# The inverse of a delta-rule scan: multiplied into keys and values per chunk, or inside each scan step

## The reference

```python
k_n = k / (norm(k) + 1e-6); state = 0
for t in range(S):
    y[t] = q[t] @ state
    state = state + beta[t] * outer(k_n[t], v[t] - k_n[t] @ state)
```

## Time and profile before

| | |
|---|---|
| time, median of 3 runs | 1041.93 us (1041.87 to 1047.24) |
| profiled execution: its own time | 1037.31 us |
| its span | 1035.6 us |
| TensorE busy with matmuls | 979.5 us (95%) |
| VectorE busy | 449.3 us (43%) |
| ScalarE busy | 167.2 us (16%) |
| GpSimd busy | 109.6 us (11%) |
| mean DMA rate | 71 GB/s |

### The profile page before, as it was taken

How to read it: one execution, slowest core, us unless ns; L and a number is a source line. 1 busy time by engine, 2 the same in 40 slices (tenths; PEclk the granted TensorE clock), 3 DMA queues, 4 the chain that set the end, 5 groups by cost and what they waited for, 6 DMA issues and landing times. The chain is left out here.

```text
span 1035.6 us, 22935 instructions
## 1 busy us (share of the span) xinstructions
PE 979.5 (95%) x10037; PEld 661.4 (64%) x10037; DVE 449.3 (43%) x1086; ACT 167.2 (16%) x352; POOL 109.6 (11%) x137
## 2 busy tenths in 40 slices
PE   6989999999999999999999999999999359999996
PEld 5875666566566566557666665666555248788785
DVE  6866753947356835734772565211011212112121
ACT  2121121120121022012102210211110011111110
POOL 4010100011010110001011001001001112212221
PEclk9989999999999999999999999999999769999998
DMA  9502003001300310040022000001900014444400
GB/s 354 234 21 89 3 17 138 2 3 35 120 3 2 108 48 2 1 154 3 1 52 104 3 1 32 18 1 18 373 22 16 32 26 158 151 158 152 153 30 27
DMA packets 29147, 74.03 MB, mean 71 GB/s; under 512 B 3944, under 2 KB 19992, under 8 KB 28160
## 3 DMA queue, kind: packets, MB, share of 16 engines
q1 hardware_dynamic: 18960, 56.74, 15.4%
q10 hardware_dynamic: 6912, 9.55, 2.6%
q0 software_dynamic: 3184, 6.39, 2.0%
HBM read 60.62 MB, written 13.00 MB: 71 GB/s over the span
## 5 line engine op out<-in xcount | busy, mean ns | idle before, releaser
L859 PE MATMUL ps<-xT,wg 128*128 128x384 f32 x576 | 208.3, 499 | 0.7 <-ACT xT L661 0.7
L879 PE MATMUL ps<-wo,prod 128*128 128x393 f32 x576 | 203.4, 501 | 2.9 <-DVE prod L558 2.9
L868 PE MATMUL ps<-xT,wv 128*128 128x384 f32 x576 | 204.6, 491 | 0.0
L558 DVE TENSOR_TENSOR prod<-sig,ps 128x384 f32<-128x384 f32 x96 | 53.2, 554 | 250.3 <-PE ps L868 249.9
L859 PEld LDWEIGHTS ps<-xT,wg 128*128 128x128 f32 x576 | 108.2, 193 | 72.0 <-issue 4.2
L879 PEld LDWEIGHTS ps<-wo,prod 128*128 128x128 f32 x576 | 105.3, 189 | 75.2 <-DVE prod L558 5.3
L868 PEld LDWEIGHTS ps<-xT,wv 128*128 128x128 f32 x576 | 107.0, 190 | 70.8 <-issue 1.3
L1131 PEld LDWEIGHTS ps_h<-xgT,arena 128*128 128x128 f32 x816 | 96.3, 196 | 5.2 <-ACT xgT L1088 1.0
L1131 PE MATMUL ps_h<-xgT,arena 128*128 128x128 f32 x816 | 96.6, 280 | 0.6 <-ACT xgT L1088 0.6
L666 ACT ACTIVATE sig<-ps 128x384 f32<-128x384 f32 x96 | 47.1, 490 | 277.1 <-PE ps L859 277.1
L1143 PE MATMUL ps_y<-arena,hT 128*128 128x384 f32 x272 | 90.5, 486 | 0.0
(11 more groups left out here) (154 smaller groups left out, 775.7 us busy)
## 6 DMA issues: line engine op xcount, KB each, us to landing
arena<-in_moe_w SPq DMA_DIRECT2D x16, 1536.0 KB, 10.6
arena<-in_kq SPq DMA_DIRECT2D x7, 1536.0 KB, 9.8
x_scratch<-x ACTq DMA_DIRECT2D x24, 196.5 KB, 4.1
arena<-in_kr SPq DMA_DIRECT2D x8, 576.0 KB, 5.3
vr<-in_v SPq DMA_DIRECT2D x8, 576.0 KB, 10.6
out<-x ACTq DMA_DIRECT2D x24, 192.0 KB, 3.2
prod<-in_turned_moe_w_out SPq DMA_DIRECT2D x1, 2304.0 KB, 11.6
wo<-in_moe_w_out SPq DMA_DIRECT2D x1, 2304.0 KB, 24.1
```

The costliest lines, as they stand in the source:

```text
L558: nc.vector.tensor_tensor(prod[:, f, :], sig[:, f % 2, :], ps_m[3 - f % 2][:, 0:CT], ALU.mult)\
L859: last = nc.tensor.matmul(ps_m[f % 2][:, 0:CT], wg[:, a, f * P:(f + 1) * P], xT[:, a, :], start=(a == 0), stop=(a == KT - 1))
L868: last = nc.tensor.matmul(ps_m[3 - f % 2][:, 0:CT], wv[:, a, f * P:(f + 1) * P], xT[:, a, :], start=(a == 0), stop=(a == KT - 1))
L879: last = nc.tensor.matmul(ps_m[t][:, 0:XW], prod[:, a, t * P:(t + 1) * P], wo[:, a, :], start=(a == 0), stop=(a == NF - 1))
```

## The change

`wu` is gone with its two evacuations. Each scan step gets a third event `apply` between `read` and `write`: `read` multiplies the bare keys with the state, VectorE takes z = V - K S in place (`z_of`), `apply` multiplies u = T z (16 matmuls of 48 columns), ScalarE copies u to a buffer `ub`, and `write` reads `ub`. The head blocks are laid so that `apply`, `write` and the query part of `gram` cross the partition halves and use all four tiles. The query part of y no longer shares PSUM columns with the score part: ScalarE copies it to `yo` after `read`, and VectorE adds the score part to `yo` after `write`. `gram` is split into 32 matmuls of 64 columns per third in place of 16 of 128.

The squares of the keys get a load of their own (`kn`, 576 KB per chunk, issued for chunk q once `from_lanes` of q - 1 is done). The first root is taken on ScalarE with four short VectorE instructions that refine it; the others stay on GpSimd. The set-up of masks is in another order, and TensorE no longer waits for it at its start. The order by hand has other fill: one dense piece more ahead of `off` 0 where preparation was still under way, `norm` of the next chunk after `off` 1, and in the prologue other `warm` counts and a later start of chunk 1's preparation.

```diff
         order += [("router", 0, 0)] + [("gram", 1, i) for i in range(3)] + [("warm", 0, 14)]     # 12 before
-    order += [("from_lanes", 0, 0), ("router_copy", 0, 0), ("off", 0, 0), ("warm", 1, 4), ("off", 0, 1)]
-    order += [("pt", 0, i) for i in range(3)] + [("warm", 1, 3), ("wu", 0, 0), ("norm", 1, 0), ("warm", 1, 2), ("wu", 0, 1),
-                                                 ("warm", 1, 2)]
-    later = prepare(1)
+    order += [("from_lanes", 0, 0), ("router_copy", 0, 0), ("off", 0, 0), ("warm", 1, 2)] + [("pt", 0, i) for i in range(3)]
+    order += [("off", 0, 1), ("norm", 1, 0), ("warm", 1, 2)]
     for step in scan(0):
+        if step[0:2] == ("apply", 1):
+            later = prepare(1)
         order.append(step)
         if step != scan(0)[-1]:
             order.append(("warm", 1, 1))
-        behind(0.5)
+        behind(0.3)
...
+            late = len(later) > 0
             while later:
                 dense(1.0)
             order.append(("from_lanes", q, 0))
-            dense(2.0)
+            dense(3.0 if late else 2.0)
             order.append(("off", q, 0))
-            if follows:
-                order.append(("norm", q + 1, 0))
             dense(1.2)
             order.append(("off", q, 1))
             dense(1.1)
-            order.append(("wu", q, 0))
-            dense(1.0)
-            order.append(("wu", q, 1))
-            dense(1.0)
             if follows:
-                order += [("gram", q + 1, 0), ("gram", q + 1, 1), ("pt", q + 1, 0)]
+                order += [("norm", q + 1, 0), ("gram", q + 1, 0), ("gram", q + 1, 1), ("pt", q + 1, 0)]
...
             elif stage == "read":                                      # VectorE
-                nc.vector.tensor_tensor(u, u, ps_a[:, 0:2, 0:W4], ALU.subtract).then_inc(u_ready, 1)
+                nc.vector.tensor_tensor(z, z, ps_a[:, 0:2, 0:W4], ALU.subtract).then_inc(z_ready, 1)
+            elif stage == "write":
+                ...  # st as before, from ps_a[:, 0:2]
+                if s % SB:
+                    dve.wait_ge(q_copied, reads(s))
+                    dve.wait_ge(y_done, s + 1)
+                    nc.vector.tensor_tensor(y, y, own_y, ALU.add).then_inc(y_copied, 1)
...
+            elif stage == "apply":                                     # ScalarE
+                act.wait_ge(u_done, s + 1)
+                nc.scalar.activation(ub[:], ps_a[:, 0:2, W4:2 * W4], ACT.Copy).then_inc(u_ready, 1)
+            elif stage == "read":
+                act.wait_ge(q_done, reads(s))
+                nc.scalar.activation(yo..., ps_a[:, 2:4, 0:W4]..., ACT.Copy).then_inc(q_copied, 1)
...
+                for a in range(2):                                     # TensorE, gram
+                    for j in range(2):
+                        for g in range(G2):
+                            for h in range(HH):
+                                n, to = ((G2 * j + g, h), (2 * G2 + HH * j + h, g))[a]
+                                for c in range(CG):
+                                    last = nc.tensor.matmul(banks[rows(to), c, n * C:(n + 1) * C], kq[part, ..., h, 0, :],
+                                                            kq[part, ..., h, a, :], start=True, stop=True)
...
+            elif stage == "apply":
+                for x in range(SEQ):
+                    for c in range(CG):
+                        for g in range(G2):
+                            for h in range(HH):
+                                last = nc.tensor.matmul(ps_a[rows(g), h, o:o + D], tt[rows(h), n, :], vr[rows(h), b, ...])
             elif stage == "write":
+                pe.wait_ge(u_ready, s + 1)
                 ...
+                for x in range(SEQ):
+                    for h in range(HH):
+                        for c in range(CG):
+                            for g in range(G2):
+                                last = nc.tensor.matmul(ps_a[rows(h), 2 + g, o:o + D], pt[rows(g), b, n, :],
+                                                        ub[rows(g), h, ...], start=True, stop=True)
```

More of the change, by code:

```diff
@@ L135, in program_order, with build @@
     return order + [("route", Q - 1, 0), ("rank", Q - 1, 0)]
[L138 removed]
+def build(nc, kq_d, kr_d, kn_d, v_d, beta_d, wg_d, wv_d, wo_d, ws_d, wgt_d, w1_d, w2_d, wo_t_d, out):
     Q = kq_d.shape[0]
@@ L444, in link @@
             dve.wait_ge(chain, links[0])
[L446 to L457, removed]
@@ L458, in _, with masks_of_rows @@
-        link(nc.vector.tensor_scalar(tri[:, 1, H2:C], tri32[:], upper[:, 0:1], lower[:, 0:1], ALU.mult, ALU.add))
+        def masks_of_rows():
+            dve.wait_ge(masks, 2)
+            link(nc.vector.reduce_sum(tri[:], tri4[:].rearrange("p h t -> p t h"), axis=AX.X))
+            nc.vector.tensor_tensor(upper[:], own[:, 0:1], own[:, 2:3], ALU.add).then_inc(consts, 1)
+            link(nc.vector.tensor_tensor(lower[:], own[:, 1:2], own[:, 3:4], ALU.add))
+            link(nc.vector.tensor_scalar(tri32[:], tri[:, 0:H2], upper[:, 0:1], None, ALU.mult))
+            link(nc.vector.scalar_tensor_tensor(out=tri32[:], in0=tri[:, H2:C], scalar=lower[:, 0:1], in1=tri32[:],
+                                                op0=ALU.mult, op1=ALU.add))
@@ L595, in _ @@
             mlp(stage, q, i)
+            if (stage, q) == ("norm", 0):
+                masks_of_rows()
+            elif (stage, q, i) == ("mask", 0, 0):
+                masks_of_scores()
     @block.scalar
     def _(act):
-        act.wait_ge(consts, 1)
+        act.wait_ge(half_ready, 1)
+        nc.scalar.activation(spare[:], half[:], ACT.Sqrt)
         def raw(q, i):
-            pair = gram_banks(q, i).rearrange("p c (n a t) -> p c n a t", n=2 * G2, a=2)
-            nc.scalar.activation(by_group(pt[:, q % 2], 2 * G2 * i, 2 * G2), pair[:, :, :, 1, :], ACT.Copy)\
-                .then_inc(raw_copied, 1)
+            scores = gram_banks(q, i)[:, :, 2 * G2 * C:].rearrange("p c (n t) -> p c n t", t=C)
+            nc.scalar.activation(by_group(pt[:, q % 2], 2 * G2 * i, 2 * G2), scores, ACT.Copy).then_inc(raw_copied, 1)
         def att(stage, q, i):
@@ L624, in att @@
                     .then_inc(upper_ready, 1)
+                if q == 0:
+                    for third in range(3):
+                        raw(0, third)
+                    nc.scalar.activation(spare[:], half[:], ACT.Sigmoid)
             elif stage == "off" and i == 0:
@@ L686, in _ @@
     def _(pe):
-        pe.wait_ge(masks, 1)
         def rows(h):
@@ L779, in att @@
                                     last = nc.tensor.matmul(
-                                        ps_a[rows(h), c, a * W4 + o:a * W4 + o + D], kq[part, b, SEQ * i + x, g, h, a, :],
-                                        st[part, h, o:o + D], start=(a == 0 and x == 0 and g == 0), stop=(a == 0),
-                                        skip_group_check=True)
-                last.then_inc(ws_done, 1)
+                                        ps_a[rows(h), 2 * a + c, o:o + D], kq[part, b, SEQ * i + x, g, h, a, :],
@@ new lines, in att @@
+                                        st[part, g, x * W2 + h * D:x * W2 + (h + 1) * D], start=True, stop=True)
+                    last.then_inc((ks_done, q_done)[a], 1)
+            elif stage == "apply":
+                s, b = q, q // JS % 2
+                if s % SB:
+                    pe.wait_ge(z_ready, reads(s))
+                else:
+                    scan_free(s // JS)
+                for x in range(SEQ):
+                    for c in range(CG):
+                        for g in range(G2):
+                            n, o = CN * c + G2 * (SEQ * i + x) + g, W4 + x * W2 + c * D
+                            for h in range(HH):
+                                last = nc.tensor.matmul(
+                                    ps_a[rows(g), h, o:o + D], tt[rows(h), n, :], vr[rows(h), b, n * D:(n + 1) * D],
+                                    start=True, stop=True)
+                last.then_inc(u_done, 1)
```

244 lines of the change are left out of this document (118 added, 126 removed).

## The result

The changed kernel takes 1002.03 us (median of 4 runs, 999.64 to 1002.23), the kernel before beside it 1042.11 us. The ratio is 0.9599, 95% interval 0.9566 to 0.9632: 4.0% faster. The forecast was 997 us with a range of 987 to 1022.

What follows compares the result with a forecast made beforehand. TensorE's work was taken to bound the mixed chunks, a chain of hand-overs the prologue. Terms of -34.5 and -9.5 make -44 us: 993 us on the profiled 1037.31, 998 against the median 1041.9; forecast 997 us, range 987 to 1022.

Steps and rivals of the forecast that it cites:

- `wu` gone: Chunks 1 to 7: 14 stages of 2.27 us plus 0.19 us excursion each disappear, -34.4 us; their evacuations return nothing.
- `apply`: Chunks 1 to 7: 21 new stages of 32 instructions at 16 ns plus 0.19 us excursion each, +14.7 us.
- y part over four tiles: In `write`, chunks 1 to 7: 21 y parts take 0.50 in place of 1.04 us, -11.3 us; the least trusted term.
- `gram`: Chunks 2 to 7: 192 instructions at 16 ns for 96 at 30, 3.07 us for 2.95, +0.7 us in all.
- waits for the transpose, and the clock after: Before `off` 0: one more MLP piece covers three waits, -4.0 us; no half clock after the longest, -1.7 us.
- new waits, stalls, clock: Mixed chunks: waits in the longer chain of a step and for `norm` on VectorE, bounds 0 and 5 us, taken as +1.5.
- mixed chunks together: Sum of all terms for chunks 1 to 7, -34.5 us.
- prologue: Up to `x_turn`: -8.5 us from `off` 0 to first `write`, -1.0 from there; -9.5 us, bounds -5 and -12.
- 64 ns per instruction and tile: Small matmuls: each tile needs about 64 ns per instruction, so what counts is how many tiles work.
- The first rival: Y part and `gram`'s query half: pairs don't overlap, two tiles idle; 11.3 us lost, 9.2 more, 1017 us; chance 0.18.
- The second rival: Prologue gives nothing: clock falls after a wait and longer steps eat the gain; +9.5 us, 1007 us; chance 0.12.
- the third: The 21 steps: `apply` or `write` waits behind VectorE's queue, then half clock; up to 3.4 us each, 1069 us; chance 0.05.

Runs made afterwards that it cites:

- e3: Changed kernel with the y part's 16 matmuls ordered by step as round of four tiles, pairs, four in a row per tile: 0.58, 0.61 and 1.38 us.
- e2b: Changed kernel with the y part on two tiles in turns, without adding up in PSUM: y part 1.04 us, first `val` piece to experts 735.87 us.
- e11: Changed kernel with chunk 0's rank later, prologue idle time filled, a step between last `val` and first `out`, other chunk 1 fill: 990.52 us, ratio 0.9516.
- e7: Changed kernel with the first root on GpSimd again, without the four refining VectorE instructions: `off` 0 at 44.68 us in both, `x_turn` 0.6 us later.
- e1: The kernel before run once more with no edit, one profiled execution: 1039.92 us.
- e9: Changed kernel with the rank of chunk 0's tokens two MLP pieces later, so GpSimd's indirect DMAs that follow move: 996.47 us, ratio 0.9564.
- e6: Changed kernel with the 16 matmuls of each `apply` issued twice: `apply` from 0.62 to 1.08 us, first `val` piece to experts 735.54 us.
- e5: Kernel before with three MLP pieces in place of two ahead of `off` 0 where preparation was still under way: ratio 0.9967, 3.4 us.

## Why the prediction was right, and by how much not

**The mechanism** was right: TensorE's sum sets the time, a small matmul costs by how many tiles work, and `wu` less `apply` and the y part are the gain. The changed kernel lies 5 us above the forecast. That it isn't further off is in part luck: the mixed chunks gave 11.1 us less than forecast on the profiled executions, the prologue 2.4 more, and the medians lie 4.6 us further apart than the two profiles. By parts, on the profiled executions (-35.5 us of span against -44 forecast):

| term | forecast | measured |
|---|---|---|
| `wu` gone | -34.4 | stages gone as read before |
| `apply` | +14.7 | 21 x (0.62 + 0.19) = +17.0 |
| y part over four tiles | -11.3 | 21 x (0.61 - 1.04) = -9.0 |
| `gram` | +0.7 | 6 x (3.21 - 2.95) = +1.6 |
| waits for the transpose, and the clock after | -5.7 | 4.1 to 0.2 us, half clock there gone |
| new waits, stalls, clock | +1.5 | `ub` 1.4, product +1.4, issue gaps and clock 3.7: +6.5 |
| mixed chunks together | -34.5 | -23.4 |
| prologue | -9.5 | -11.9 |

The measured terms, with -34.4 and -5.6 for the first and fifth, add up to -23.9.

**The excursion's end.** I priced `apply` and the new y part by the state part of `write`, 0.50 us. But that stage is followed by another of the same kind. By the single starts, the 32 instructions start within 0.46 us in all three; the next small stage then starts 0.04 us after the last of them, an MLP piece 0.15. So the last small stage of an excursion keeps 0.11 us more to its end: 0.61 and 0.62 in place of 0.50. That is 2.3 us in each of the two terms: right mechanism, size off. The prediction's 64 ns per instruction and tile hid it, for the old y part's 1.04 us is 16 starts on each tile 58 ns apart and such an end.

**Pairs of tiles** overlap, as the order of starts in the earlier trace rows suggested: e3 shows 0.61 against 0.58, and that three instructions can wait at a tile. The prediction said that three or more can and that the new order needs exactly three; that is just at the limit. The Trainium skill, "TensorE: Matmul & The Clock Gate", Part 3, would have matmuls start strictly in program order; e3's 1.38 in place of 2 us for four in a row contradicts it for these tiles. e2b confirms the price of two tiles, 1.04. The first rival falls.

**New waits.** The prediction gave them 1.5 us and named VectorE's queue. None of that came. What came was in three places. For `ub` the queue was ScalarE's: the copy of an output tile and the issue of its two DMAs stood in front.

```profile
134.09 0.68 PE L800 MATMUL ps<-vr,tt 64*64 64x48 f32 x32
134.19 0.50 ACT L698 ACTIVATE x<-ps 128x393 f32<-128x393 f32 x1 [1.66 <-PE ps L902]
134.72 0.40 ACTq L701 DMA_DIRECT2D out<-x  x1
135.16 0.45 ACTq L702 DMA_DIRECT2D x_scratch<-x  x1
135.65 0.49 ACT L670 ACTIVATE ub<-ps 128x384 f32<-128x384 f32 x1 [0.95 <-PE ps L800]
```

It is the one place that the prediction named as standing with no piece between, but it counted only the copy. The product of the last `val` is waited for six times in place of four: in chunks 3 to 7 and the last one `out` now follows `val` directly, before it did so in chunks 2, 3, 4 and the last one. With a step put between them, in e11, all but one of these waits go. The third place is the issue stall, which no row of the one profile before could show.

**The clock.** The half clock at 289 us is gone with its wait, as forecast; another, behind the stall at 229 us, took its place in this execution, so the clock was not at 1.00 throughout from 90 us on, as the prediction had it.

**The prologue.** `off` 0 started at 44.68 us (45.4 forecast), and `x_turn` at 63.53 where 66 was forecast. From the first `write` (51.24) to `x_turn` 12.3 us passed, where 13.9 was forecast; the clock stayed at 1.00 from 44 to 62 us, so 1.6 of the 2.7 us set aside for it came back and other waits took the rest. (The prologue's own terms add up to 9.75, not 9.5.) e7 shows that TensorE's own work ahead of `off` 0 set its start. The second rival falls, and so does the third.

**Which execution is the base.** The profile of before that carried the sum had none of the stalls (1037.31 us against the median of 1042), that of after had one. On the spans the gain is 35.5 us, on the medians 40.1. The luck is in the base: e1 is the same kernel with 3.9 us of stalls, while the changed kernel's stall stands in every profile that has its order there. A comparison of the first two profiles alone would have put the whole difference on the change.

**What is open.** What holds up TensorE's instructions. e9 shows that moving the indirect DMAs away from that `read` removes the stall, not what they share with it; the same DMAs stood beside the same y parts in the first profile of before (the second one at 440.83 us, a y part from 440.77 on) without a gap, and the gap in e6's prologue came without any. Whether the prologue's filled idle time keeps the clock up in every execution wasn't settled.

## What to carry to other kernels

Price small matmuls by the busiest tile: 58 ns here for each instruction that it gets; orders in pairs of tiles are enough, four matmuls in a row on one tile are not. Add a fixed 0.3 us for each excursion between dense pieces (0.19 in the piece, 0.11 at the stage's end), so two short stages in two places cost more than one. When a copy joins a chain between engines, count all that its queue holds in front of it, the issue of DMAs too.

## What the runs showed of the hardware

- Matmuls of different 64x64 tiles start out of program order; three instructions can wait at a tile, and a fourth holds the ones behind it (e3: 0.58, 0.61 and 1.38 us for the same 16 matmuls; in the last the next tile starts at 240 ns, just after the fifth of eight at 234).
- One tile starts an instruction of 48 columns every 58 ns; with four tiles that is one every 14 to 15 ns on average (e6: 32 more in 0.46 us).
- From the last start of a small stage to the next matmul it takes 0.04 us if that is small too and 0.15 if it is of the full array (`write` and the piece behind it).
- TensorE's supply of instructions can stall in steps of 0.7 us (gaps of 0.4) in stages of small matmuls, nearly always while GpSimd issues indirect DMAs: none and five gaps in the two profiles of the kernel before, eight in e5, two or three in one `read` in all eight profiles with the changed kernel's order there, none when the DMAs were moved (e9), one in e11. One gap, in e6's prologue, had no such DMA near it.
